# Expert layer: the down products of a tile issued two tiles behind its up products, with one tile instead of four transposed by TensorE

## The reference, cut to what matters

```python
top2 = np.argpartition(-noisy_logits, 2, axis=1)[:, :2]
top2_w = softmax over the two chosen logits
for e in range(E):
    for k in range(2):
        mask = top2[:, k] == e
        h = np.maximum(x[mask] @ w1[e], 0.0)                       # up, relu
        out[mask] += top2_w[mask, k, None] * (h @ w2[e])           # down
```

## Time and profile before

| | us |
|---|---|
| median of 3 runs | 990.65 (989.6, 990.65, 993.1) |
| the profiled execution, whole | 996.31 |
| its span, first to last instruction | 994.7 |
| PE busy in it | 957.5 (96%) |
| DVE / ACT / POOL busy | 520.5 / 322.0 / 516.1 |
| mean granted TensorE clock | 0.989 |

### The profile page before, as it was taken

How to read it: one execution, slowest core, us unless ns; L and a number is a source line. 1 busy time by engine, 2 the same in 40 slices (tenths; PEclk the granted TensorE clock), 3 DMA queues, 4 the chain that set the end, 5 groups by cost and what they waited for, 6 DMA issues and landing times.

```text
span 994.7 us, 18458 instructions
## 1 busy us (share of the span) xinstructions
PE 957.5 (96%) x5864; PEld 845.6 (85%) x5865; DVE 520.5 (52%) x942; ACT 322.0 (32%) x446; POOL 516.1 (52%) x743
## 2 busy tenths in 40 slices
PE   6999999999999999999989999989999899999996
PEld 6989999999999999999767788867888678888884
DVE  5554555556556556563756554544455345444354
ACT  3322233243242242332313333333333233333231
POOL 5996000100200200598668868788588859803355
PEclk9999999999999999999989999999999999999998
DMA  8352142342342242654657767666676774448639
GB/s 337 124 196 75 38 143 75 96 149 75 94 151 75 88 125 97 191 191 147 199 168 175 159 167 172 170 137 157 146 177 180 158 179 95 95 95 166 182 107 317
DMA packets 193896, 145.99 MB, mean 147 GB/s; under 512 B 159921, under 2 KB 160049, under 8 KB 193841
## 3 DMA queue, kind: packets, MB, share of 16 engines
q1 hardware_dynamic: 175360, 89.94, 35.8%
q0 software_dynamic: 12288, 44.05, 14.5%
q10 hardware_dynamic: 6192, 11.27, 3.0%
HBM read 65.80 MB, written 40.63 MB: 107 GB/s over the span
## 4 chain that ended last, share of the span: by engine, by line
PE 72%; POOL 14%; DMA 5%; DVE 4%; issue 2%; SPq 1%; ACT 1%; POOLq 1%; ACTq 0%; DVEq 0%
PE ps L1330 18%; PE ps L1432 17%; PE ps L1317 16%; PE ps L1344 12%; PE ps L1348 6%; POOL W L506 5%; DMA hT_halves<-h_halves 4%; POOL W L553 3%; POOL W L503 3%; POOL y_hi L594 2%; PE ps L1358 1%; POOL W L549 1%; DMA Wraw<-w_moe 1%; PE ps L1286 1%; PE ps L1265 1%
## 5 line engine op out<-in xcount | busy, mean ns | idle before, releaser
L1432 PE MATMUL ps<-W,hT_part 128*128 (+1 forms) x1032 | 252.2, 400 | 12.3 <-DVE hT_part L1214 10.4
L1317 PE MATMUL ps<-W,xg_part 128*128 (+1 forms) x1032 | 251.4, 398 | 4.2 <-DVE xg_part L977 4.2
L1432 PEld LDWEIGHTS ps<-W,hT_part 128*128 128x128 f32 x1032 | 197.0, 192 | 61.2 <-issue 15.3
L1317 PEld LDWEIGHTS ps<-W,xg_part 128*128 128x128 f32 x1032 | 194.6, 189 | 51.5 <-issue 4.7
L1330 PE MATMUL ps<-x_part,W 128*128 128x384 f32 x1152 | 222.0, 341 | 3.4 <-POOL W L506 2.9
L1330 PEld LDWEIGHTS ps<-x_part,W 128*128 128x128 f32 x1152 | 200.7, 188 | 6.7 <-POOL W L506 4.8
L553 POOL TENSOR_TENSOR W<-EXraw,W 128x256 fp32r<-128x256 f32 x224 | 190.7, 882 | 4.7
L516 POOL DMA_INDIRECT routed_x<-x_halves,slot_blk x30 | 29.6, 988 | 293.3 <-DVE slot_blk L932 284.7
L1344 PE MATMUL ps<-g_part,W 128*128 128x384 f32 x768 | 150.6, 338 | 0.0
L1344 PEld LDWEIGHTS ps<-g_part,W 128*128 128x128 f32 x768 | 134.8, 188 | 0.3 <-ACT g_part L638 0.2
L549 POOL TENSOR_SCALAR W<-EXraw 128x256 fp32r<-128x256 f32 x224 | 108.5, 510 | 39.1 <-PE ps L1317 32.1
(11 more groups left out here) (180 smaller groups left out, 743.5 us busy)
## 6 DMA issues: line engine op xcount, KB each, us to landing
EXraw<-in_w POOLq DMA_DIRECT2D x24, 1024.0 KB, 6.7
QKV<-qkv SPq DMA_DIRECT2D x15, 768.0 KB, 4.5
routed_y<-y_sb ACTq DMA_DIRECT2D x43, 256.0 KB
routed_y<-zero_tile SPq DMA_DIRECT2D x14, 768.0 KB, 4.0
Wraw<-w_moe SPq DMA_DIRECT2D x16, 512.0 KB, 8.3
EXraw<-in_w SPq DMA_DIRECT2D x8, 1024.0 KB, 5.6
out<-y_lo SPq DMA_DIRECT2D x18, 256.0 KB
routed_x<-zero_tile SPq DMA_DIRECT2D x8, 256.0 KB, 2.1
```

Source lines behind the costliest of these rows:

```text
L1317: last = nc.tensor.matmul(dst, a(ha), b(hb), start=(opens and i == 0), stop=(closes and i == n - 1))
L1432: last = nc.tensor.matmul(ps[:, 4, :], hT_part[hh][:, n, :], W[hw][:, weights(slot, W1W + n * DM, DM)], start=(n == 0 and k == 0), stop=(n ...
```

## The change

- TensorE's loop issues up(g) and then down(g-2), for g = 4 to 41. It begins with up(3) and up(4) without a down product between them. At the end come up(42), down(40), down(41), down(42).
- DMA transposes now serve tiles 3 to 41. Only tile 42 goes through TensorE (in the middle of down(40)), with buffers `h_last` and `hT_last` of its own. The residual matmuls and the negative identity are gone; DVE takes the low part.
- In ACT's and DVE's loops turned_high and turned_low of tile g-1 now stand before merge of tile g; take_y and store_y are those of g-2.
- Tile 41's split is done in two halves of four blocks (`end_high`, `end_low`), the first as soon as half of down(40) is done. Tiles 40, 41, 42 have a PSUM bank each for y (`y_bank`), and DVE copies them.
- In `tile_tables` the row table comes first, with a semaphore of its own (`row_ready`) for SP.
- The rank matmuls inside down(0) come at block 3 instead of 4.

The first `turned_tile` in the diff is ACT's, the second DVE's.

```diff
-        LAST = 3
-        GL = G - LAST
+        GL = G - 1
+        def y_bank(g):
+            return 4 + g - (GL - 2) if isinstance(g, int) and g >= GL - 2 else 4
...
-            sp.wait_ge(tab_ready, 1)
+            sp.wait_ge(row_ready, 1)
...
-            with sp.Fori(EARLY + 1, GL - 1) as g:
+            with sp.Fori(EARLY + 1, G - EARLY) as g:
                 for s in range(2):
                     turn_half(g, s)
                 turn_x(g + EARLY)
-            turn_x(G - 1)
+            for g in range(G - EARLY, GL):
+                for s in range(2):
+                    turn_half(g, s)
...
             def turned_tile(g, first=False):
                 halve(g, first)
                 xg_high(g + 1)
+                if not first:
+                    turned_high(g - 1)
+                    store_y(g - 2)
                 merge(g)
-                turned_high(g)
-                store_y(g - 1)
...
-            for g in range(GL - 1, G):
-                if g > GL:
-                    hidden_rest(g - 1)
-                hidden(g)
-                if g + 1 < G:
-                    xg_high(g + 1)
-                if g > GL:
-                    copy_y(g - 1)
-                store_y(g - 1)
-                hidden_high(g)
-            hidden_rest(G - 1)
-            copy_y(G - 1)
-            store_y(G - 1)
+            hidden(GL)
+            end_high(GL - 1, 0)
+            hidden_high(GL)
+            end_high(GL - 1, 1)
+            for g in range(GL - 2, G):
+                store_y(g)
...
+            def turned_tile(g, first=False, more=True):
                 halve(g, first)
                 xg_low(g + 1)
-                merge_x(g + 2)
+                if more:
+                    merge_x(g + 2)
+                if not first:
+                    take_y(g - 2)
+                    turned_low(g - 1)
                 merge(g)
-                take_y(g - 1)
-                turned_low(g)
...
-            xg_low(GL)
-            merge_x(GL + 1)
+            turned_tile(GL - 1, more=False)
+            end_low(0)
+            hidden_low(GL)
             take_y(GL - 2)
-            hidden_low(GL - 1)
-            xg_low(GL + 1)
-            merge_x(GL + 2)
+            end_low(1)
             take_y(GL - 1)
-            xg_low(GL + 2)
+            take_y(GL)
...
             expert_up(EARLY, tell=True)
-            expert_down(EARLY - 1)
-            with pe.Fori(EARLY + 1, GL - 1) as g:
+            with pe.Fori(EARLY + 1, GL) as g:
                 expert_up(g, turned=True, tell=True)
-                expert_down(g - 1)
-            pe.wait_ge(minus_ready, 1)
-            for g in range(GL - 1, G):
-                expert_up(g, between=(lambda g=g: h_residual(g - 1)) if g > GL else None, turned=g == GL - 1)
-                expert_down(g - 1)
-                hidden_transpose(g)
-            h_residual(G - 1)
-            expert_down(G - 1)
+                expert_down(g - 2)
+            expert_up(GL, turned=True)
+            expert_down(GL - 2, between=lambda: hidden_transpose(GL))
+            expert_down(GL - 1)
+            expert_down(GL)
```

More of the change, by code:

```diff
@@ L176, in attention_moe_moe_program @@
         hT = place("hT", [P, KF, P], F32, XP1_AT)
+        h_last = place("h_last", [P, F2], F32, X1T_AT)
+        hT_last = [place(f"hT_last{c}", [P, KF, P], F32R, (X1_AT, X1H_AT)[c]) for c in (HI, LO)]
         half_bytes = 2 * BANK * 2
@@ L674, in hidden @@
                 if g >= EARLY:
-                    act.wait_ge(hh_ready, g)
-                    act.wait_ge(hl_ready, g)
-                nc.scalar.activation(h_sb[:], ps[:, 0:2, :].rearrange("p a b -> p (a b)"), ACT.Relu).then_inc(h_taken, 1)
+                    for s in range(2):
+                        act.wait_ge(halves_turned[s], 16 * (GL - EARLY))
+                nc.scalar.activation((h_sb if g < EARLY else h_last)[:], ps[:, 0:2, :].rearrange("p a b -> p (a b)"), ACT.Relu).then_inc(h_taken, 1)
             def store_y(g):
@@ L684, in hidden_high @@
                 act.wait_ge(hT_in_psum, by_engine(g))
-                nc.scalar.copy(hT_part[HI][:], ps[:, 2:4, :].rearrange("p a (n c) -> p (a n) c", c=P)).then_inc(hh_ready, 1)
+                src = ps[:, 2:4, :].rearrange("p a (n c) -> p (a n) c", c=P)
+                if g < EARLY:
+                    nc.scalar.copy(hT_part[HI][:], src).then_inc(hh_ready, 1)
+                else:
+                    nc.scalar.copy(hT_last[HI][:], src).then_inc(last_hi, 1)
             def layer_block(i, par, w3, base, gate, attend):
@@ L1386, in up_half, with expert_up @@
                 return product(ps[:, s, :], terms, range_of_k[0] == 0, range_of_k[-1] == KD - 1)
-            def h_residual(g):
-                pe.wait_ge(hh_ready, g + 1)
-                for a in range(2):
-                    last = nc.tensor.matmul(ps[:, 2 + a, :], minus[:], hT_part[HI][:, 4 * a:4 * a + 4, :].rearrange("p n c -> p (n c)"),
-                                            start=False, stop=True, skip_group_check=True)
-                last.then_inc(h_rest, 1)
-            def expert_up(g, between=None, turned=False, tell=False):
+            def expert_up(g, turned=False, tell=False):
                 slot = expert_slot(g)
@@ L1402, in expert_up @@
                 for s in range(F2 // BANK):
-                    if s > 0 and between is not None:
-                        between()
                     if turned:
@@ L1423, in expert_down @@
                     pe.wait_ge(ex_down_ready, need)
-                pe.wait_ge(hh_ready, g + 1)
-                pe.wait_ge(hl_ready, g + 1)
-                if not isinstance(g, int) or g > 0:
+                static = isinstance(g, int)
+                rows = hT_last if static and g == GL else hT_part
+                if static and g == GL:
+                    pe.wait_ge(last_hi, 1)
+                    pe.wait_ge(last_lo, 1)
+                elif not static or g < GL - 1:
+                    pe.wait_ge(hh_ready, g + 1)
+                    pe.wait_ge(hl_ready, g + 1)
+                if not static or 0 < g <= GL - 2:
                     pe.wait_ge(y_taken, g)
                 for n in range(KF):
-                    if between is not None and n == KF // 2:
+                    if between is not None and n == at_n:
                         between()
+                    if static and g == GL - 1 and n % (KF // 2) == 0:
+                        pe.wait_ge(end_hi, n // (KF // 2) + 1)
+                        pe.wait_ge(end_lo, n // (KF // 2) + 1)
                     for k, (hh, hw) in enumerate(PASSES):
-                        last = nc.tensor.matmul(ps[:, 4, :], hT_part[hh][:, n, :], W[hw][:, weights(slot, W1W + n * DM, DM)],
+                        last = nc.tensor.matmul(ps[:, y_bank(g), :], rows[hh][:, n, :], W[hw][:, weights(slot, W1W + n * DM, DM)],
                                                 start=(n == 0 and k == 0), stop=(n == KF - 1 and k == 2))
+                    if static and g == GL - 2 and n == KF // 2 - 1:
+                        last.then_inc(down_half, 1)
                 last.then_inc(y_ready, 1)
```

68 lines of the change are left out of this document (40 added, 28 removed).

## The result

The changed kernel took **1003.54 us** (median of 4 runs, 1001.4 to 1003.9), the kernel before 991.57 beside it (4 runs, 989.6 to 993.1). The ratio is 1.0106, 95% interval 1.0059 to 1.0153: about 1% slower, outside my range of 984 to 994. The profiled execution took 1003.38, its span is 1001.5 us, and the mean granted clock fell from 0.989 to 0.979.

The account below looks back on a forecast made before the run. TensorE bounds the loop (15.4 us of late hidden tiles); gathers and last sums bound the end. The span falls 3.3 us, 994.7 to 991.4; from median 990.65 that gives 987.3, plus 1.4 for late tiles 988.7; range 984 to 994.

Parts of the forecast that it names:

- The loop: TensorE's expert loop with down(g-2): hidden-tile waits cost nothing, 11.3 us won later on, down(39) ends at 944.5.
- The gaps at the start: TensorE waits 2.3 us before up(4) and 1.9 before up(5); of the first 4.1 us only 0.4 is won.
- I take nothing: Lower clock after the two start gaps: up to 2.4 us more each was possible, none was charged.
- Undisturbed, 18 gathers at 1.25 are issued by 970.6: Last gathers on POOL: out before most of the scalings; if held, issued until 979 and no gain, 994.7.
- TensorE's end: 968.0: TensorE's last product, down(42), ends at 968.0 where before TensorE stopped at 987.5.
- My third rival: Slower, 994.5, chance 0.16: end is TensorE's end + 23.4 us; 5.7 late tiles and 4.0 low clock give 997.
- So 988.2, and 3.2 to the end: 991.4: End of span: take_y, scalings 7.2 and sums 12.1 after TensorE's end give 988.2, span 991.4 against 994.7.
- I take a quarter: Of the 5.7 us between profiled execution and median, 1.4 is late tiles lost from the gain: 988.7.
- the upper bound I gave, 993.0: Time if all of the 5.7 us between profiled execution and median is late tiles; 987.3 if none.

Follow-up runs that it names:

- e9: The changed kernel run again unedited, on another chip than the first measurement's or possibly the same; 992.26 us, 1.0027 against the kernel before.
- e17: The changed kernel unedited, a fourth time, as the control for e18 on the same chip; 1002.28 us, 1.0106 against the kernel before.
- e14: The changed kernel unedited, a third time, on yet another chip; 1002.63 us, 1.0102 against the kernel before.
- e18: The changed kernel with at most two of the last 18 gathers in flight; 1001.82 us, 1.0107 against the kernel before.
- e6: The changed kernel with WARM_LONG (warm-up matmuls per group in the prologue) 12 instead of 16; 991.81 us, 1.0007 against the kernel before.
- e2: The changed kernel with WARM_LONG (warm-up matmuls per group in the prologue) 4 instead of 16; 992.31 us, 1.0042 against the kernel before.
- e10: The changed kernel with WARM_LONG (warm-up matmuls per group in the prologue) 20 instead of 16; 991.90 us, 1.0017 against the kernel before.
- e13: The kernel before, unedited, profiled once more; 989.95 us, 0.9995.
- e7: The changed kernel with the last 18 gathers waiting for the store of y(40) instead of y(39); 996.85 us, 1.0072 against the kernel before.
- e12: The changed kernel with ScalarE copying y of tiles 40 to 42 and scaling y_lo, and result_rows behind xg_low of tiles 5 and 6; 983.04 us, 0.9920.

## Why the prediction was wrong

By its own steps:

- **The loop**: right. No wait for a hidden tile is left in it; down(39) ended at 944.9 for 944.5. POOL's waits for a down product grew (12.7 us in five, the longest 5.8) and stayed hidden.
- **The gaps at the start**: right in place and size (2.20 and 2.09 us for 2.3 and 1.9); in the later profiles the first is up to 3.6 and the second can be gone (e9: 3.59 and 0.56; e17: 3.58 and none). "I take nothing" for the lower clock held in the first profile; in e9 and e14 the up product behind the first gap took 7.40 and 7.25 us for 5.85, in e17 and e18 8.58 and 8.48, so this gap often costs 1.4 to 2.7 more.
- **"Undisturbed, 18 gathers at 1.25 are issued by 970.6"**: right here, 971.9 and none over 0.95; on a clean chip the last ones come under the scalings and can be held (e9 below). That is where the argument stopped too soon. I asked what VectorE does to the gathers and what the gathers do to the outputs, never what they do to TensorE.
- **"TensorE's end: 968.0"**: the step that failed, 978.8. I summed TensorE's products at their undisturbed length and took its signals as prompt, beside 18 gathers. The 10.8 us are paid almost whole (span 1001.5 for 991.4), because the change has put VectorE's 36 instructions behind TensorE's last product. Of the 14.8 us between forecast and median 10.4 lie here; the other 4.4 are two points further down. My third rival had the place right and the cause wrong: it looked for the loss in late tiles (5.7) and in the low clock behind the two gaps (4.0), and came to 997.
- **"So 988.2, and 3.2 to the end: 991.4"**: right where TensorE isn't slowed. The spans of e6, e2 and e10 are 991.0, 991.3 and 989.7, and 22.7 of the 23.4 us behind TensorE's end are also in the slowed run.
- **"I take a quarter"** of the 5.7 us as late tiles: wrong. By e13 it is most of it, near the upper bound I gave, 993.0. On the clean chips the changed kernel and its neighbours in WARM_LONG took 991.8 to 993.0.

So there are two results. Where the chip isn't disturbed by the gathers, the change is worth nothing or costs some tenths of a per cent (e9: 1.0027 [0.9999, 1.0054]): by my sum, the late tiles it removes are paid back by up(41) ahead of the last real tile and by VectorE's place. Where it is, the change costs 1.0% (three measurements: 1.0106, 1.0102, 1.0106). The Trainium skill, "SBUF — State Buffer", section "Who interferes with whom", was right that VectorE's scalings can hold a gather: in e9 the last but one gather came under them and took 5.63 us on POOL. The last took 11.66 us and lay under the sums (974.25 to 985.60), each of which reads two tiles in SBUF; from an operation with two such inputs (`tensor_tensor`) the section infers no harm to the writing of descriptors, and here the measurement decides. Nor is every gather beside the scalings held: in e7 five in a row took 1.2 to 1.3 us.

## What to carry to other kernels

An edit that frees a stream of transfers from what held it back has a second price: whatever runs beside that stream now, and whatever has been moved to stand behind it. Work on the path that ends the kernel is best tied to the last product that it needs, not to the last product there is: with the scalings on an engine that does not hold the gathers, that and one table moved took the changed kernel from 992.3 to 983.0 on one chip (e9, e12). And before one explains a stretch that was seen once, run the same kernel again on another chip; five experiments went into a place in the program, and none of them ran on a chip that slows. A profiled execution 5.7 us above the median must be asked what it lost them to before a saving is charged against it.

## What the hardware showed that I had not expected

- A dense stream of indirect gathers (1.25 us apart, 207 GB/s from 958 to 966 us in e17) delays TensorE's signals, by 2.8 and 11.0 us in the first profile, 13.6 in e14 and 8.8 in the control, and stretches some of its register instructions from 32 and 46 ns to 700. It does so on some chips only: in the first measurement and on two chips of the five after it. It ends 3.0 to 3.5 us after the last gather is issued. Two gathers in flight (e18: about 2 us apart, 171 GB/s) don't do it.
- It isn't the load of the DMA engines as such. In e17 their share was 0.76 from 958 to 966 while TensorE was nearly idle (0.43 us busy of 8). In e9, on a chip that isn't disturbed, it was 0.84 with TensorE busy throughout; and in e13, on e14's chip, which does slow, outputs and gathers together made 0.88 and 303 GB/s with TensorE busy throughout and clean. The rows of the window table, e17:

```profile
958.00:966.00 8.00, 0.43 (x3) 0.07 (x1) 1.38 (x2) 0.63 (x1) 5.87 (x8) 0.74 0.76 207
```

e9:

```profile
958.00:966.00 8.00, 8.00 (x36) 6.46 (x35) 0.69 (x1) 0.00 (x0) 5.92 (x7) 1.00 0.84 264
```

and e13:

```profile
962.00:970.00 8.00, 8.00 (x36) 6.48 (x35) 5.39 (x9) 2.05 (x2) 7.09 (x4) 1.00 0.88 303
```

- The time of a gather on POOL beside VectorE's work varies widely: 0.95 us undisturbed, 1.2 to 1.3 beside the scalings in e7, 5.63 beside them in e9 and 11.66 beside its sums. Three of e9's twelve runs took 995.8 to 996.5, the others 990.6 to 993.2; the profiled one was of the three, with both gathers held.
